# Reordering the last steps of an attention prologue on five engines, and storing the last output tile in two halves

## The reference

```python
for t in range(S):
    cur = einsum('bhd,bhe->bhde', u * k[t], v[t])
    y[t] = einsum('bhd,bhde->bhe', r[t], state + cur)
    state = w * state + einsum('bhd,bhe->bhde', k[t], v[t])
```

## Time and profile before

| | |
|---|---|
| median of 3 runs | 864.23 us (863.23 to 864.37) |
| the profiled execution's own time | 864.19 us |
| its span, first to last instruction | 862.7 us |
| TensorE busy | 856.3 us, 99% of the span |
| VectorE, ScalarE, GpSimd busy | 505.5, 377.6, 180.3 us |
| share of TensorE in the chain that ended last | 99% |
| data moved by DMA | 56.6 MB, 66 GB/s over the span |

### The profile page before, as it was taken

The page is one execution under the profiler, slowest core; times in us unless marked ns, Lnnn a source line. Parts: engine busy times, 40 slices in busy tenths (PEclk is TensorE's granted clock), DMA queues, the critical chain, the costliest instruction groups (busy, mean ns, idle before and its releaser), DMA issues.

```text
span 862.7 us, 14214 instructions
## 1 busy us (share of the span) xinstructions
PE 856.3 (99%) x6253; PEld 709.9 (82%) x6253; DVE 505.5 (59%) x522; ACT 377.6 (44%) x394; POOL 180.3 (21%) x116
## 2 busy tenths in 40 slices
PE   8999999999999999999999999999999999999998
PEld 7888888888888888888888888888888888888886
DVE  6897766765676765554369554454554554554443
ACT  4687766566656556666697221121121121220211
POOL 3762334433334442200236200000000000000000
PEclk9999999999999999999999999999999999999999
DMA  7644331122123212102223110110110000100100
GB/s 277 199 159 159 105 139 62 63 89 63 55 94 115 58 63 89 64 2 83 88 78 128 56 36 1 37 37 0 37 38 1 36 1 1 37 0 1 38 1 36
DMA packets 19633, 56.62 MB, mean 66 GB/s; under 512 B 2928, under 2 KB 4976, under 8 KB 19568
## 3 DMA queue, kind: packets, MB, share of 16 engines
q1 hardware_dynamic: 14544, 44.74, 15.5%
q10 hardware_dynamic: 5024, 10.95, 3.6%
HBM read 44.28 MB, written 9.44 MB: 62 GB/s over the span
## 4 chain that ended last, share of the span: by engine, by line
PE 99%; DVE 1%; issue 0%; ACT 0%; POOL 0%; DVEq 0%; POOLq 0%
PE y_ps L862 45%; PE h_ps L805 34%; PE a_ps L805 11%; PE a_ps L666 2%; PE a_ps L643 1%; PE a_ps L656 1%; PE h_ps L631 1%; PE y_ps L673 1%; PE y_ps L805 0%; DVE tables L1140 0%; PE h_ps L686 0%; PE a_ps L710 0%; PE y_ps L710 0%; PE y_ps L715 0%; PE a_ps L715 0%
## 5 line engine op out<-in xcount | busy, mean ns | idle before, releaser
L805 PE MATMUL h_ps<-x_split,win_hi 128*128 128x512 f32 (+1 forms) x864 | 265.8, 389 | 0.0
L862 PE MATMUL y_ps<-g_hi,wout_lo 128*128 128x512 f32 x576 | 224.1, 389 | 0.0
L862 PE MATMUL y_ps<-g_hi,wout_hi 128*128 128x512 f32 x576 | 224.1, 389 | 0.0
L862 PE MATMUL y_ps<-g_lo,wout_hi 128*128 128x512 f32 x576 | 224.1, 389 | 0.0
L805 PEld LDWEIGHTS h_ps<-x_split,win_hi 128*128 128x128 f32 x864 | 159.9, 188 | 33.2 <-issue 0.2
L805 PE MATMUL h_ps<-x_split,win_lo 128*128 128x512 f32 (+1 forms) x432 | 167.0, 387 | 0.0
L1202 DVE TENSOR_TENSOR g_lo<-mid,g_hi 128x1024 fp32r<-128x1024 f32 x96 | 143.9, 1498 | 3.3
L1209 DVE TENSOR_TENSOR mid<-mid 128x1024 f32<-128x1024 f32 x48 | 61.1, 1274 | 136.5 <-ACT mid L979 136.5
L862 PEld LDWEIGHTS y_ps<-g_hi,wout_hi 128*128 128x128 f32 x576 | 108.1, 188 | 22.5
L862 PEld LDWEIGHTS y_ps<-g_hi,wout_lo 128*128 128x128 f32 x576 | 108.1, 188 | 22.4
L862 PEld LDWEIGHTS y_ps<-g_lo,wout_hi 128*128 128x128 f32 x576 | 108.1, 188 | 22.4
(11 more groups left out here) (135 smaller groups left out, 825.0 us busy)
## 6 DMA issues: line engine op xcount, KB each, us to landing
att<-in_att SPq DMA_DIRECT2D x20, 584.0 KB, 5.8
att<-in_att SPq DMA_DIRECT2D x20, 512.0 KB, 3.7
w_raw<-in_w_in SPq DMA_DIRECT2D x16, 384.0 KB, 3.1
w_raw<-in_w_out SPq DMA_DIRECT2D x16, 384.0 KB, 3.1
x_dram<-mid ACTq DMA_DIRECT2D x6, 768.0 KB, 3.3
att<-x_dram SPq DMA_DIRECT2D x6, 768.0 KB, 4.4
out<-mid ACTq DMA_DIRECT2D x5, 768.0 KB, 3.9
mid<-in_first_T SPq DMA_DIRECT2D x2, 512.0 KB, 4.5
```

The costliest lines, as they stand in the source:

```text
L805: m = nc.tensor.matmul(ps, a, b_, start=n == 0, stop=n == len(terms) - 1)
L862: m = nc.tensor.matmul(y_ps[:, o, :], a, b_, start=unit == 0 and t == 0 and j == 0, stop=unit == UNITS - 1 and t == 1 and j == 2, skip_gro ...
```

## The change

There are five edits in the order and one in the last store.

1. TensorE: `keep_warm` is 2, 1 and 1 in place of 5 and 3; the last one stands behind `first_own(1)`.
2. TensorE: `first_product(0, half=0)` is issued ahead of `first_main(2)` and `first_main(3)`; half 1 comes behind `first_states(3)`.
3. GpSimd: block 0's low part is made ahead of `fill_odd(3)`, and the wait for `early_T` at 4 is gone.
4. VectorE: `decay_first_k(3)` stands ahead of `mask_first(3)`.
5. The last tile is copied as two halves of 256 columns, which both count a new semaphore `last_halves`. SyncE stores the first half, ScalarE the second.

```diff
@@ sync
+            sp.wait_ge(last_halves, 1)
+            sp.dma_start(out[:, KT - 1, (GROUPS - 1) * GROUP:(GROUPS - 1) * GROUP + 256], y_sb[:, KT - 1, 0:256])\
+              .then_inc(out_stored, 16)
             sp.wait_ge(x2_stored, 16 * GROUPS)
-            sp.wait_ge(out_stored, 16 * (GROUPS - 1 + KT))
+            sp.wait_ge(out_stored, 16 * (GROUPS + KT))
@@ gpsimd
                 first_product(2)
                 first_product(3)
-                fill_odd(3)
-                pool.wait_ge(early_T, PER)
                 raw, hi, lo = w_views(0)
                 pool.wait_ge(w_hi_done, 1)
                 pool.tensor_tensor(lo, raw, hi.bitcast(f32), ALU.subtract).then_inc(w_first_done, 1)
+                fill_odd(3)
                 decay_T(PER)
@@ tensor
-            keep_warm(5)
+            keep_warm(2)
             first_own(0)
-            keep_warm(3)
+            keep_warm(1)
             first_own(1)
+            keep_warm(1)
@@ tensor
             first_item_scores(3)
+            first_product(0, half=0)
             first_main(2)
             first_main(3)
-            first_product(0, half=0)
             first_states(2)
+            first_states(3)
             first_product(0, half=1)
-            first_states(3)
             item_scores(PER)
@@ scalar
-                    for o in range(KT):
+                    for o in range(KT - 1):
                         act.wait_ge(y_tile, o + 1)
                         act.activation(y_sb[:, o, :], y_ps[:, o, :], ACT.Copy).then_inc(y_free, 1)
                         act.wait_ge(y_free, G + 1 + o)
                         act.dma_start(out[:, o, g * GROUP:(g + 1) * GROUP], y_sb[:, o, :]).then_inc(out_stored, 16)
+                    act.wait_ge(y_tile, KT)
+                    for half in range(2):
+                        cols = slice(half * 256, (half + 1) * 256)
+                        act.activation(y_sb[:, KT - 1, cols], y_ps[:, KT - 1, cols], ACT.Copy).then_inc(last_halves, 1)
+                    act.wait_ge(last_halves, 2)
+                    act.dma_start(out[:, KT - 1, g * GROUP + 256:(g + 1) * GROUP], y_sb[:, KT - 1, 256:])\
+                       .then_inc(out_stored, 16)
                     return
@@ vector
             decay_first_k(2)
             mask_first(2)
+            decay_first_k(3)
             mask_first(3)
             first_x_lo(2)
-            decay_first_k(3)
             first_x_lo(3)
```

More of the change, by code:

```diff
@@ L246, in attention_mlp @@
         x2_hi_done, x2_done = sem("x2_hi_done"), sem("x2_done")
+        last_halves = sem("last_halves")
         block = ctx.enter_context(nc.Block())
```

## The result

| | before | changed |
|---|---|---|
| median of 6 runs each | 864.04 us (863.23 to 865.07) | 867.07 us (865.71 to 869.74) |
| ratio | | 1.0037, 95% interval 1.0021 to 1.0053 |
| profiled execution: time, span | 864.19, 862.7 us | 869.74, 868.2 us |

The kernel got slower by 3.0 us, 0.37%; 863.4 with 862.5 to 864.9 was forecast. The profiled execution is the slowest of the six, 5.55 us over that of before, so its sizes are larger than those of the median.

What follows compares the result with a forecast made beforehand. TensorE, 99% of the chain, was taken as the bound: time falls only where its sequence shortens or idle stretches go. 864.19 less 0.5 (kept ahead of W = 1) and 0.25 (end) gave about 863.4 us, range 862.5 to 864.9.

Steps and rivals of the forecast that it cites:

- Fewer idle products: TensorE's start: three fewer products let `first_own(0)` start at 6.81; all up to item 3's scores 0.5 us earlier, bounds 0 and 0.75.
- rival 3: Start of TensorE: clock rises later, narrow products and transposes cost double, all behind shifts 1.3 us; 865.2 to 866.3; chance 0.08.
- Half 0 ahead of the values: TensorE, items 2 and 3: half 0 covers the idle 0.69 us; with the early 0.5, `item_scores(4)` is reached 1.11 us earlier.
- Rival 2: SyncE's wait for item 2's values: late loads decide, W = 1 starts 0.66 late; 864.6, up to 865.1; chance 0.14.
- What is late next: Up to W = 1: loads of u, block 3 and block 7 let 0.5 of 1.11 us stay; 0.6 becomes a wait.
- The end: Last tile's copy and store in two halves: net gain 0.25 us, bounds 0.34 and a loss of 0.1.
- The sum: Whole kernel: 864.19 - 0.5 - 0.25 = 863.44, about 863.4 us.

Runs made afterwards that it cites:

- order-only kernel: Kernel before with only the TensorE, GpSimd and VectorE order edits, idle products and last store as before: 864.79 us against 864.24, ratio 1.0003.
- the halves too: Changed kernel with the idle products of before put back (5 and 3), order edits and halved last store kept: 864.42 us against 864.24, ratio 1.0008.
- The cut experiments: GpSimd's item 6 operations cut to a sixteenth or eighth of columns: changed kernel with products back 863.25 us, kernel before 863.92, against 863.79.
- 5, 1 and 1: Changed kernel with 5 idle products ahead of `first_own(0)`, 1 ahead of and 1 behind `first_own(1)`: 864.54 us against 863.71, ratio 1.0014.

## Why the prediction was wrong

**Fewer idle products: this step failed.** I booked 0.5 us of gain. The starts were right: `first_own(0)` at 6.61 and 6.89 in the two profiles, forecast 6.81. The clock was not. It was rival 3, to which I gave 0.08, with the argument that narrow products and idle stretches later on did not lower the clock. They didn't, in a kernel whose idle products had brought the clock up first; here the block of wide products ended at 6.1 to 7.1 us, 1.5 us after the clock's rise in one profile and 7.3 ahead of it in the other.

The sizes in rival 3 were near: 1.58 us for the narrow products at the lower level, measured 1.50 to 1.81; a delay of 1.3 for the transposes, measured 0.9 and -0.1, and 2.4 and 1.7 for the end of item 0's scores. It missed the form: the clock also fell after it had risen (at 8.0 us, up again at 18.3, in one profile; at 8.7 and 12.1 in another), and this caught the scores and the values of items 0 and 1, which cost more than the transposes. I had put it at 865.2 to 866.3; the median is 867.07. The Trainium skill (TensorE: Matmul & The Clock Gate, Part 1) has sustained activity as what releases the clock, at a moment that varies; the traces agree, with first rises from 4.6 to 14.4 us over the profiles. Read as more than a rival's footnote it would have changed the likeliest case.

What the sum had at nothing, and no rival had at all, is the wait inside `item_main(6)`, 1.25 to 1.32 us in three of the four profiles with two idle products ahead of `first_own(0)`, right behind a late block of instructions.

**Half 0 ahead of the values: right up to W = 0, and worth nothing.** TensorE reached W = 0 1.35 us earlier in the order-only kernel and 1.37 with the halves too, of which some 0.8 came with an earlier rise of the clock in those executions (transposes at 9.55, not 10.34), luck of the execution and not of the edit. The 0.6 that is left is what was forecast for the order. The idle stretch went, as forecast; u was issued at 25.68 and block 3 converted at 30.04, 0.34 earlier than before, so the loads behind item 2's values did not bind. Rival 2 named the right outcome with the wrong place.

**What is late next: the second step that failed.** I let 0.5 of 1.11 us through. None came through: W = 1 started 0.16 and 0.56 late. I had placed the limit in ScalarE's wait for block 7. It was item 6's first part. My sentence was that a chunk load comes 1.1 us earlier and clears the queue for block 7; in fact, issued 1.4 us earlier it ran into blocks 5 and 6 and landed 1.3 us later. The changed kernel has this too, though TensorE is late there: the load stands 1.44 us behind block 6 and takes 6.1, and W = 0 to W = 1 is 12.17 us where before it was 10.52. So `item_main(5)` waited 0.7 to 1.1 us for GpSimd, GpSimd's 7 us of work lay over another stretch of VectorE's, and that made the g of W = 1 late by a further 0.6 to 0.7. I held VectorE's durations for constants. They are not, and not in the order of before either: the same four operations took 5.1 us in the profile of before, 6.2 with the halves alone and 7.6 with the idle products alone, and W = 1 still started within 0.2 us of its place. What is new is that TensorE comes to W = 1 earlier than they allow. The cut experiments show this by taking the cause away.

**The end: right, somewhat smaller.** 0.25 forecast, 0.15 to 0.2 by the rows.

**The sum.** By the ratios the products alone cost 0.28% (2.4 us, with 0.5 to 4.3 in the interval), the order 0.03% (0.3), and the halves bring 0.02% (0.2): 2.5 us of 3.0, within the intervals. By the medians it is 1.16 + 0.55 - 0.27 = 1.4 us. In the changed order the products cost more than alone: 3.0 against 0.2 with them back, 2.8 us. The difference of 1.6 is near the 1.3 of the wait inside `item_main(6)`, which the profile with the products alone changed doesn't have. How often the executions without a profile have it isn't known.

**Open.** Of the 1.80 us between W = 2 and W = 3 of the changed kernel 1.25 are the wait behind the late instructions. The rest lies mostly ahead of `item_main(6)` and fits VectorE's state decay of item 5, which ended at 70.71 while TensorE began at 70.92. What makes the block of instructions late wasn't tried; more or fewer instructions ahead of that place would be the test. What the clock wants was not measured either. The times with 5, 1 and 1 say only that three wide products at this place decide over most of the loss; they do not separate the clock from the late block.

## What to carry to other kernels

Products that compute nothing can be load-bearing: before removing them, look at when the clock rose in the profile and what follows them until the first dense stretch, and try it in several executions, since one profile shows one of several outcomes. A gain in a stage is real only beyond the next place where all engines meet; shift every transfer with it and ask into which other one it now runs. When one engine's work moves against another's, their durations are not constants. And a wait that no semaphore explains is worth a look at the queue that brings the instructions.

## What was not expected of the hardware

- With the idle products alone changed, TensorE was busy for 2.90 of the 3.00 us from 5 to 8, much of it with narrow products and their weight loads, and the granted clock still fell to the 1.2 GHz level at 8.7 us. In the changed kernel it was down from 8.0 to 18.3 us.
- In another execution of the changed kernel it did not rise for 12.8 us from the first product on. A mean granted clock of 1.000 for that execution hid it; only the durations showed it.
- In three profiles TensorE stood still for 1.25 to 1.32 us at the same place of its stream, 0.1 to 0.2 us after a block of 16 KB of instructions had come, the first for about 19 us; in the nine others blocks came 7 to 14 us apart there.
- With GpSimd at work beside it, VectorE's subtraction of 128x768 took 1.75 us and not 0.95, its state decay 2.22 and not 0.56.
- A load of 512 KB that was issued 1.4 us earlier landed 1.3 us later, in 6.4 us in place of 3.7.
